# Three orders changed in the preparation stage of an attention and mixture kernel

## The reference

```python
# attention, 2 x 8 heads of 768 tokens x 64; only pairs in the same hash bucket count
q_bits = (np.einsum('bhsd,dk->bhsk', q, proj) > 0)      # 6 bits; k_bits likewise
q_bucket = np.sum(q_bits * powers, axis=-1)
mask = q_bucket[:, :, :, None] == k_bucket[:, :, None, :]
scores = np.where(mask, scale * np.matmul(q, k.transpose(0, 1, 3, 2)), -1e9)
attn = softmax(scores);  x = attn @ v                   # -> 1536 tokens x 512
# gated layer
h = ((x @ w1) * (x @ w2)) @ w3;  x = h @ w_out          # w3 1024x1024, w_out 1024x512
# mixture of 4 experts
p = domain_probs / (domain_probs.sum(-1, keepdims=True) + 1e-09)
out += p[:, e:e + 1] * (np.maximum(x @ w1[e], 0.0) @ w2[e])
```

## Time and profile before

| | us |
|---|---|
| median of 3 runs | 986.05 (985.76 to 987.55) |
| profiled execution, whole | 985.06 |
| its span | 983.3 |
| PE busy in the span | 972.8 (99%) |
| DVE, ACT, POOL busy | 601.1, 455.2, 357.3 |
| mean granted clock of PE | 0.998 |

### The profile page before, as it was taken

The page is one execution under the profiler, slowest core; times in us unless marked ns, Lnnn a source line. Parts: engine busy times, 40 slices in busy tenths (PEclk is TensorE's granted clock), DMA queues, the critical chain, the costliest instruction groups (busy, mean ns, idle before and its releaser), DMA issues.

```text
span 983.3 us, 15635 instructions
## 1 busy us (share of the span) xinstructions
PE 972.8 (99%) x5357; PEld 903.4 (92%) x5357; DVE 601.1 (61%) x961; ACT 455.2 (46%) x844; POOL 357.3 (36%) x348
## 2 busy tenths in 40 slices
PE   8899999999999999999999999999999999999998
PEld 6689999999999999999998988989989899898997
DVE  5659999999986781678754362543534535255342
ACT  4248888888885561554541331413304234042230
POOL 0113645657574320335262250522604216043130
PEclk9999999999999999999999999999999999999999
DMA  7536777775554430201110201102010011100102
GB/s 212 147 90 139 211 202 204 210 179 129 120 153 145 127 113 1 84 30 44 44 44 1 65 22 43 28 16 65 23 43 21 21 53 32 41 25 21 43 20 110
DMA packets 95058, 81.63 MB, mean 83 GB/s; under 512 B 33952, under 2 KB 78368, under 8 KB 95008
## 3 DMA queue, kind: packets, MB, share of 16 engines
q1 hardware_dynamic: 95008, 80.98, 29.6%
HBM read 54.69 MB, written 7.39 MB: 63 GB/s over the span
## 4 chain that ended last, share of the span: by engine, by line
PE 96%; SPq 2%; DVE 1%; POOL 0%; DMA 0%; issue 0%; ACT 0%; POOLq 0%
PE ps L339 24%; PE ps L338 24%; PE ps L340 24%; PE ps L1577 6%; PE ps L1564 4%; PE ps L1592 3%; PE ps L1594 3%; PE ps L1566 3%; SPq L485 1%; PE ps L1543 1%; PE ps L1525 1%; PE ps L1531 1%; PE ps L1534 1%; DMA raw_v<-in_v 0%; SPq L347 0%; DVE expo L1140 0%
## 5 line engine op out<-in xcount | busy, mean ns | idle before, releaser
L737 POOL TENSOR_TENSOR v_sum<-kept,kept 128x384 f32<-128x384 f32 x48 | 48.9, 1020 | 353.8 <-ACT kept L898 353.8
L898 ACT COPY kept<-ps 128x384 f32<-128x384 f32 x144 | 68.5, 479 | 213.2 <-PE ps L340 212.3
L1438 DVE SCALAR_TENSOR_TENSOR acc<-ps,gate,acc 128x512 f32<-128x512 f32 (+1 forms) x97 | 72.2, 744 | 140.3 <-PE ps L340 140.3
L340 PE MATMUL ps<-v_hi,hid_lo 128*128 128x512 f32 (+1 forms) x388 | 150.3, 387 | 0.0
L339 PE MATMUL ps<-v_lo,hid_hi 128*128 128x512 f32 (+1 forms) x388 | 150.2, 387 | 0.0
L338 PE MATMUL ps<-v_hi,hid_hi 128*128 128x512 f32 (+1 forms) x388 | 150.1, 387 | 0.0
L1286 DVE TENSOR_TENSOR u_sum<-ps,kept 128x384 f32<-128x384 f32 x48 | 26.8, 557 | 122.6 <-PE ps L340 122.5
L1140 DVE TENSOR_SCALAR_CACHE_REDUCE expo<-ps 128x768 f32<-128x768 f32 x96 | 91.7, 956 | 13.9 <-PE ps L1566 10.4
L829 ACT ACTIVATE expo<-expo,neg_max 128x768 f32<-128x768 f32 x96 | 90.5, 943 | 7.9 <-DVE expo L1140 5.9
L1154 DVE TENSOR_TENSOR pT_lo<-ps,pT_hi 128x768 fp32r<-128x768 f32 x96 | 90.5, 948 | 3.6 <-ACT pT_hi L843 3.2
L843 ACT CAST pT_hi<-ps 128x768 fp32r<-128x768 f32 x96 | 76.7, 800 | 24.9 <-PE ps L1577 24.6
(11 more groups left out here) (169 smaller groups left out, 2377.8 us busy)
## 6 DMA issues: line engine op xcount, KB each, us to landing
w_raw<-gate_sums SPq DMA_DIRECT2D x16, 512.0 KB, 3.6
e_raw<-in_moe_w SPq DMA_DIRECT2D x64, 128.0 KB, 2.3
v_raw<-in_moe_w SPq DMA_DIRECT2D x32, 256.0 KB, 3.1
w_raw<-in_moe_w SPq DMA_DIRECT2D x48, 128.0 KB, 3.5
made_raw<-in_moe_w SPq DMA_DIRECT2D x16, 256.0 KB, 3.7
gate_sums<-made SPq DMA_DIRECT2D x8, 512.0 KB, 2.7
raw_qk<-in_q SPq DMA_DIRECT2D x16, 192.0 KB, 3.1
raw_qk<-in_k SPq DMA_DIRECT2D x16, 192.0 KB, 3.5
```

Of the source, the lines that this page charges most:

```text
L340: return nc.tensor.matmul(out_ps, lhs_lo, rhs_hi, start=False, stop=stop, skip_group_check=onto)
L737: nc.gpsimd.tensor_tensor(v_sum[:, :], kept[s][1][:, :], kept[s][2][:, :], ALU.add).then_inc(v_done, 1)
L898: nc.scalar.copy(kept[s][n][:, :], ps[4 * s + n][:, 0:HALF]).then_inc(kept_done, 1)
L1438: nc.vector.scalar_tensor_tensor(acc[:, t, cols], down_bank(h, t, n)[:, cols], gate_f[:, bass.ds(t * E + e, 1)], acc[:, t, cols], ALU.mult ...
```

## The change

Four edits, all of order; no instruction is added to the work or taken away.

- Transfers (SP): the first halves of w3's tiles 0 and 1 are both issued ahead of the first piece of w_out. Head 0's raw v goes ahead of proj, the codes and their scalars; `domain_probs` goes behind the pieces of w3's tile 4 and head 1's q and k, and has a semaphore of its own.
- PE: in tiles 3, 5 (and 4 and 6, where the table has a step there), the second preparation step stands behind the tile's third product instead of in front of its first.
- DVE and ACT: their sides of that second step stand behind the split of the next tile (`w3T_low`, `w3T_high`).
- DVE: the mixing weights are taken out of `constants()` in tile 2 and made in tile 6.

```diff
@@ transfers
-            load_first_w3(0, 0)
-            load_wout(0)
-            load_first_w3(1, 0)
-            for kt in range(1, 4):
+            for it in range(2):
+                load_first_w3(it, 0)
+            for kt in range(4):
                 load_wout(kt)
...
             load_w3(3)
+            load_v(0, 0, True)
             sp.dma_start(proj_f[0:DH, :], proj).then_inc(const_loaded, 16)
...
+            load_w3(4)
+            load_qk(0, 1, True)
             for b in range(B):
                 sp.dma_start(dp[:, b * TILES:(b + 1) * TILES, :],
                              probs[b * S:(b + 1) * S, :].rearrange("(p t) e -> p t e", t=TILES))\
-                    .then_inc(const_loaded, 16)
-            load_w3(4)
-            load_v(0, 0, True)
-            load_qk(0, 1, True)
+                    .then_inc(probs_loaded, 16)
             load_v(0, 1, True)
@@ ACT
                 first_copy(2 * it - 2)
                 wp_high(it - 1)
-                first_copy(2 * it - 1)
                 if it < FK - 1:
                     w3T_high(it + 1, (it + 1) % 2)
+                first_copy(2 * it - 1)
@@ DVE
-                dve.wait_ge(const_loaded, 16 * (4 + B))
+                dve.wait_ge(const_loaded, 16 * 4)
...
+            def mixing_weights():
+                dve.wait_ge(probs_loaded, 16 * B)
                 nc.vector.reduce_sum(dp_sum[:, :], dp[:, :, :], axis=AX_X).then_inc(gate_step, 1)
...
-                first_code(2 * it - 1)
                 if it < FK - 1:
                     w3T_low(it + 1, (it + 1) % 2)
                 if it == 2:
                     constants()
+                if it == FK - 2:
+                    mixing_weights()
+                first_code(2 * it - 1)
                 if it + 2 < FK:
                     turn_w3(it + 2, it % 2)
@@ PE
                 first_prep(2 * it - 2)
                 if it < FK - 1:
+                    multiply_wp(it, it % 2, range(3))
                     first_prep(2 * it - 1)
+                    multiply_wp(it, it % 2, range(3, FK))
                 else:
                     pe.wait_ge(w3T_lo_done, 2 * FK)
-                multiply_wp(it, it % 2, range(FK if it < FK - 1 else FK - 2))
+                    multiply_wp(it, it % 2, range(FK - 2))
```

More of the change, by code:

```diff
@@ L245, in build_program @@
               ps45[:, 0, :], ps45[:, 1, :], ps6[:, 0, :], ps7[:, 0, :]]
-        const_loaded = sem("const_loaded")
+        const_loaded, probs_loaded = sem("const_loaded"), sem("probs_loaded")
         stage_loaded = [sem(f"stage_loaded{n}") for n in range(FK)]
```

## The result

| | before | after |
|---|---|---|
| median, 6 executions each on one chip | 986.14 us (983.98 to 988.09) | 980.66 us (980.41 to 981.53) |
| ratio after to before | | 0.9944, 95% interval 0.993 to 0.9958 |
| profiled execution | 985.06 us, span 983.3 | 981.53 us, span 979.7 |
| last matmul of tile 2 starts | 28.35 | 30.46 |
| code product of tile 4 starts | 40.86 | 38.24 |

The change makes the kernel 5.48 us faster; 980.5 was forecast.

What follows compares the result with a forecast made beforehand. PE, with 96% of the chain of waits, was taken to bound the kernel. 4.7 us up to tile 4 plus 0.8 in tile 5 gave 5.5 us, so 980.5 against the 986.05 median; range 978.5 to 983.6.

Steps and rivals of the forecast that it cites:

- v ahead of the constants: End of tile 2: raw v lands at 20.7, q_main and q_cross are ready before PE wants them; constants' delay costs nothing.
- What is late next: Tile 3: POOL's q_cross holds DVE's w3T_lo 1.5 us; PE waits 0.9 before the projection instead of 3.29 in three waits.
- The rival without a hold: Tile 3: DVE isn't held by q_cross, no PE wait is left; gain 6.4 us, 979.7; chance 0.15.
- The clock: Tile 3, 30 to 40 us: a 0.9 us gap alone is harmless, so the 2.3 us lost at lower clock are gained.
- rival 2: Clock falls all the same, at the 0.9 us gap or near the start; 2.3 us given back, 982.8; chance 0.15.
- The code product behind the third product: Tile 3: bits is in time by 0.6 us, its 0.65 wait gone; tile 4 starts at 36.2, 4.7 us earlier.
- Tile 5: Tiles 5 and 6: three products cover the 0.57 us wait between transpose groups; gain 0.8 (0.57 to 0.9), tile 6 nothing.
- w3 ahead of w_out: Kernel start: exchanged loads only move PE's 1.8 us wait to another owner; worth 0, bounds -0.8 and +0.8 us.

Runs made afterwards that it cites:

- experiment 4: Changed kernel with DVE's constants placed ahead of tile 3's w3T_lo instead of behind it: 980.78 us, ratio 0.9944 to the kernel before.
- experiments 3: Kernel before with only the second preparation step moved behind a tile's third product on PE, ACT and DVE: 982.38 us, ratio 0.996.
- experiment 2: Kernel before with only head 0's raw v loaded ahead of the constants: 984.08 us, ratio 0.9983.
- experiments 9 to 12: Four kernels on one chip: changed 981.64 us; w3/w_out exchange undone 979.78; constants ahead of w3T_lo 980.28; both (the twelfth) 978.5; kernel before 986.79.
- experiment 6: Changed kernel with five more matmuls on zeros behind the transposes of tile 1's first half: 980.51 us, ratio 0.9935 to the kernel before.
- experiment 1: Changed kernel with the first w3 and w_out transfers back in the old order: 979.9 us, ratio 0.9939 to the kernel before.
- experiment 5: Kernel before with only the first w3 halves loaded ahead of w_out: 988.58 us, ratio 1.0012.
- experiment 7: Changed kernel with the mixing weights made in tile 2 again, behind the constants: 981.61 us, ratio 0.9944 to the kernel before.

## Why the prediction was right, and where it was not

**v ahead of the constants: right.** v landed 2.9 us after its issue (taken: 3.8), POOL's split began at 19.86 (forecast near 21), and q_main and q_cross were ready before PE wanted them. q_cross ended at 28.63, not before 27 as I had written, since tile 2 came 2.11 us later. Neither the constants' nor w3's transfers were missed.

**What is late next: right in mechanism and nearly in size.** DVE's w3T_lo was forecast at 2.7 us and took 2.55; PE's wait at 0.9 and was 0.56, 0.72 with the restart (30.46 + 0.23 to 31.41). The rival without a hold falls by the rows of the same w3T_lo in the changed kernel and in experiment 4: 2.55 beside POOL's q_cross and 1.23 once it is over. My wording was too narrow, though: I named pairs of two-input operations, and experiments 3 and 4 show small casts (2.40 for 0.75) and a one-input addition (1.55 against 0.17 in experiment 2) held as well. The Trainium skill ("SBUF — State Buffer", "Who interferes with whom") counts VectorE's casts and scalar operations among those that can contend, when they run in its two-port modes. The two rows agree with that if these instructions ran in such a mode, which no row here shows.

**The clock: right in tile 3, not at the start.** A gap of 0.56 did it no harm, and rival 2's 2.3 us were not given back in tiles 3 and 4. Experiments 2 and 3 bound it from the other side: in the same stretch, 0.41 and then 2.17 us in one piece were followed by the pace of 0.43, while 0.73, 0.82 and 0.42 with matmuls between were not. Rival 2 had named the start of the kernel as well, and there PE did spend 4.12 us more at half clock; that is the failed step below.

**The code product behind the third product: right.** Experiment 2 shows what it is for: without it the early v leaves a wait of 2.17 for bits. With the two edits together the stretch is 7.78, where the sum said 7.85 (28.35 to 36.2). From the same start, the forecast for tile 4's code product, 36.2, becomes 38.31 with tile 2's delay of 2.11; it was 38.24. For tile 6's first projection, 50.0 becomes 52.11; it was 52.13.

**Tile 5: right.** From tile 5's first transposes to tile 7's code product, 13.46 before (46.52 to 59.98) and 12.69 after (43.91 to 56.60): 0.77, forecast 0.8.

**w3 ahead of w_out: the step that failed.** "The wait changes its owner" was right, "I take 0" was not, and the bound of 0.8 does not hold either: by experiments 9 to 12 the exchange costs 1.8 us. I had counted the shift of the two landings alone and left out PE's clock behind them. In the two profiles shown, the first product comes only 0.23 us later (7.76 and 7.99). But the pace of 0.43 lasts 4.12 us longer (9.98 to 14.10), which is some 9.6 matmuls at 0.20 us more for each, 1.9; with the 0.23 that is the 2.11 us by which tile 2 ends later. How long the slow pace lasts varies from profile to profile, and the two orders nearly part: it lasts until 10.87 to 14.10 in the six with the exchange and without zeros; in the seven without the exchange, until 9.42 to 11.59 in five and not at all in two (experiments 2 and 12). That PE's standing still in front of the products has to do with it is supported by experiment 6, one profile against those six. Why a wait of the same length costs less with the transposes behind it than with the products behind it is only argued: the transposes are then work for PE directly ahead of the products. The length of the wait alone doesn't decide it; in experiment 1 it was 2.0 us, and PE began at 0.23, fell to 0.43 and was up again at 11.59.

**Why the total fits all the same.** From profile to profile the sum closes with the missing term: 985.06 less 5.5 for the stretch and tile 5, and 2.1 more for the start, is 981.7; the changed kernel's profiled execution took 981.53. But that one is 0.9 above its median, and the kernel before's is 1.1 below its own. These two offsets, 2.0 us, stand against the term I had missed, and by the medians the forecast came out exact. The forecast knew only the second as 1.0. With the missing 1.8 us in the sum it would have been 982.3, 1.6 above the median. The kernel before scatters widely (983.72 to 989.78 on one chip, the changed one 980.48 to 983.01). The mean granted clock of its executions says more. Of the 53 that ran beside the experiments, 26 had 0.998, as the profiled one, and a median of 984.96 us; 27 had 0.994 to 0.997 and a median of 987.46. No execution of the changed kernel is below 0.998, and against those like the profiled one on the chip of experiments 9 to 12 (984.67) it gains 3.0 us (981.64), near the 3.5 of the two profiles. So about half of the kernel before's executions lose more than its profile shows, and the change takes that loss away as well. Where it lies is open: that these executions have a later v, or waits for k_main as in experiment 5, is only argued, since none of them was seen in a profile. The sum had neither this gain nor the cost of the exchange; that the two are of one size, so that the total came out exact, is luck.

## What to carry to other kernels

When a late transfer holds up an engine, look at which engine comes next in line and move its part too: here v alone gave about 2 us, the order of the steps alone about 4, and with both of them the waits in this place are down from 3.3 to 0.6 us. Where two loads are exchanged at the start of a kernel, follow both consumers up to the first matmul that needs both. Here it mattered what PE did directly ahead of its long run of matmuls, since each of them took 0.43 us at half clock instead of 0.23. Where VectorE works beside a long GpSimd instruction, look at what stands between the held instruction and the result that the busiest engine waits for: here, w3T_lo (1.23 us) taken from that place shortened the stretch by 0.8 us.

## What the runs showed that I had not expected

- The granted clock's column can read 1.00 for the first 20 us while the matmuls start 0.43 us apart (until 14.10 in the changed kernel). Early in a kernel the pace has to be read from the starts.
- With matmuls on zeros in the gap in front of the first product, the pace of 0.43, which lasted until 14.10 us, was not there; but PE then waited 1.68 us for w3's tile 3, whose pieces also came late in that execution (experiment 6).
- The end of tile 2 lies between 27.56 and 30.69 us in the profiles of this case. With the exchange it is 28.77 to 30.69 in seven profiles, without it 27.56 to 29.07 in seven: the spread within an order is nearly as large as what the order is worth, which is why one profile of each could not show it.
- One profiled execution lost 3.4 us in waits for k_main in the attention (experiment 5) and another 1.6 (experiment 7), where the other twelve lost 0.2 to 0.7. Neither edit touches that place.
